# Splitting weights inside the attention loops: an edit of load order, waits and TensorE's tile order

## The reference, cut to what matters

```python
# 1: q, k, v [2, 8, 768, 64]; chunks of 32 queries, 16 keys to the left, 8 to the right, 8 memory keys
for c in range(nc):
    k_full = np.concatenate([mem_k, k_ctx], axis=2)
    scores = scale * np.matmul(q_c, k_full.transpose(0, 1, 3, 2))
    scores = scores - np.max(scores, axis=-1, keepdims=True)
    a = np.exp(scores)
    a = a / (np.sum(a, axis=-1, keepdims=True) + 1e-09)
    out[:, :, c_start:c_end] = np.matmul(a, v_full)
# 2: mix, x [2, 768, 512], w_k [512, 1024], w_v [1024, 512], w_r [512, 512]
xk = mu_k * x + (1.0 - mu_k) * x_prev
xr = mu_r * x + (1.0 - mu_r) * x_prev
k = np.maximum(xk @ w_k, 0.0)
v = k * k @ w_v
x = v / (1.0 + np.exp(-(xr @ w_r)))
# 3: each token goes to one of 8 experts, chosen by its own logits or by the token before it
h = np.maximum(x[b, s] @ w1[e], 0.0)
out[b, s] = p[e] * (h @ w2[e])
```

## Time and profile before

| | |
|---|---|
| median of three runs | 531.41 us (528.64 to 531.82) |
| the profiled execution, its own time | 533.26 us |
| its span | 531.5 us |
| TensorE busy, matmuls | 440.0 us, 83% |
| TensorE busy, weight loads | 366.4 us, 69% |
| VectorE busy | 245.9 us, 46% |
| ScalarE busy | 212.7 us, 40% |
| GpSimd busy | 55.3 us, 10% |
| chain that ended last | PE 67%, DMA 14%, issue 7%, DVE 5%, POOL 3%, ACT 2% |
| first mix matmul | 82.91 us |

### The profile page before, as it was taken

How to read it: one execution, slowest core, us unless ns; L and a number is a source line. 1 busy time by engine, 2 the same in 40 slices (tenths; PEclk the granted TensorE clock), 3 DMA queues, 4 the chain that set the end, 5 groups by cost and what they waited for, 6 DMA issues and landing times.

```text
span 531.5 us, 10141 instructions
## 1 busy us (share of the span) xinstructions
PE 440.0 (83%) x3759; PEld 366.4 (69%) x3759; DVE 245.9 (46%) x477; ACT 212.7 (40%) x319; POOL 55.3 (10%) x62
## 2 busy tenths in 40 slices
PE   1667628999999999999940069999999999999993
PEld 1545518889898989989830047777777777777772
DVE  2454575653535234354045149222382247464861
ACT  1333474663435253344022038222462245555750
POOL 0000000010100101010003601111111111111110
PEclk9967867999999999999975569999999999999998
DMA  8668442428000000000004779511173128383810
GB/s 302 253 208 294 157 181 86 152 90 309 0 0 0 0 0 0 0 0 1 2 0 158 238 281 406 209 54 40 52 227 136 40 71 253 141 251 132 271 61 10
DMA packets 18313, 67.31 MB, mean 127 GB/s; under 512 B 2734, under 2 KB 2734, under 8 KB 18288
## 3 DMA queue, kind: packets, MB, share of 16 engines
q1 hardware_dynamic: 13104, 50.92, 27.9%
q0 software_dynamic: 4896, 16.05, 8.8%
q10 hardware_dynamic: 288, 0.02, 0.0%
HBM read 55.41 MB, written 12.62 MB: 128 GB/s over the span
## 4 chain that ended last, share of the span: by engine, by line
PE 67%; DMA 14%; issue 7%; DVE 5%; POOL 3%; ACT 2%; SPq 1%; POOLq 0%; DVEq 0%; ACTq 0%
PE PS L530 16%; PE PS L403 12%; PE PS L513 12%; PE PS L435 10%; DMA QK<-tiles 5%; PE PS L419 5%; DMA XR<-grouped_rows 5%; POOL grouped_rows L1107 2%; PE PS L521 2%; PE PS L453 2%; PE PS L504 1%; PE PS L330 1%; PE PS L357 1%; DMA RAW<-wmix 1%; PE PS L343 1%
## 5 line engine op out<-in xcount | busy, mean ns | idle before, releaser
L1022 DVE TENSOR_TENSOR ELO<-ERAW,EHI 128x1024 fp32r<-128x1024 f32 x56 | 66.8, 1219 | 12.9 <-ACT EHI L696 10.3
L696 ACT ACTIVATE EHI<-ERAW 128x1024 fp32r<-128x1024 f32 x56 | 57.4, 1053 | 29.6 <-DMA ERAW<-wexp 20.8
L403 PE MATMUL PS<-XHI,WHI 128*128 128x256 f32 x192 | 56.6, 295 | 1.2 <-DVE WLO L805 1.2
L530 PE MATMUL PS<-EHI,HH 128*128 128x512 f32 x128 | 54.6, 426 | 2.6 <-issue 1.0
L403 PE MATMUL PS<-XHI,WLO 128*128 128x256 f32 x192 | 55.2, 287 | 0.0
L403 PE MATMUL PS<-XLO,WHI 128*128 128x256 f32 x192 | 55.1, 287 | 0.0
L513 PE MATMUL PS<-EHI,XSH 128*128 128x512 f32 x128 | 53.0, 414 | 1.4 <-DVE XSL L1030 1.4
L1043 DVE TENSOR_TENSOR HL<-PS,HH 128x512 fp32r<-128x512 f32 x32 | 22.1, 691 | 66.3 <-ACT HH L716 65.9
L513 PE MATMUL PS<-ELO,XSH 128*128 128x512 f32 x128 | 51.5, 402 | 0.0
L513 PE MATMUL PS<-EHI,XSL 128*128 128x512 f32 x128 | 51.2, 400 | 0.0
L530 PE MATMUL PS<-EHI,HL 128*128 128x512 f32 x128 | 50.6, 395 | 0.0
(11 more groups left out here) (141 smaller groups left out, 774.6 us busy)
## 6 DMA issues: line engine op xcount, KB each, us to landing
ERAW<-wexp SPq DMA_DIRECT2D x56, 512.0 KB, 5.6
QK<-tiles SPq DMA_DIRECT2D x12, 768.0 KB, 5.7
VV<-tiles SPq DMA_DIRECT2D x12, 520.0 KB, 3.9
grouped_rows<-ZR POOLq DMA_DIRECT2D x1, 5140.0 KB, 18.1
RAW<-wmix SPq DMA_DIRECT2D x10, 512.0 KB, 3.8
XR<-grouped_rows POOLq DMA_DIRECT2D x17, 257.0 KB, 4.2
CO<-consts SPq DMA_DIRECT2D x1, 470.0 KB, 6.5
rows_out<-OSB,OIDX POOLq DMA_INDIRECT x16, 3.9
```

What stands on the lines that cost most here:

```text
L403: last = nc.tensor.matmul(PS[q % 2][:, half * 256:half * 256 + 256], w[:, c:c + P], x[:, k, :], start=n == 0, stop=n == 11)
L530: last = nc.tensor.matmul(PS[4][:, :], x[:, f, :], ww[:, c:c + D], start=n == 0, stop=n == 23)
L696: nc.scalar.activation(EHI[w][:, c * CH2:(c + 1) * CH2], ERAW[c][:], ACT.Copy).then_inc(ehi_done, 1)
L1022: nc.vector.tensor_tensor(ELO[w][:, c * CH2:(c + 1) * CH2], ERAW[c][:], EHI[w][:, c * CH2:(c + 1) * CH2].bitcast(F32), ALU.subtract).then_ ...
```

## The change

All ten chunks are loaded, and split, inside the attention loops: SP loads chunk t at the end of `ahead(t)`, behind the QK load of tile t+4 and a wait for `weight_lo` of chunk t-2 (`wlo_done` starts at 2, so that the first two don't wait and every later count is higher by 2). ScalarE does `weight_hi(t-2)` at the end of tile step t, VectorE `weight_lo(t-2)` behind `normed(t)`, in all pairs but the first. The mix layer holds none of them any more.

The waits for the V and QK loads move from `probs_transposed` to `values` and `scores`. TensorE's tile order becomes probabilities(t), x(t-1), values(t), scores(t+2). Each of the two gets an increment of a semaphore, `passed_pe`, that no engine waits for.

`CO` is loaded in two parts: the identity where the whole was loaded, the tables behind the last chunk, with a semaphore of their own; `X2R`'s token column is filled from them in mix pair 0.

```diff
-            sp.dma_start(CO[:], consts).then_inc(const_in, 16)
+            sp.dma_start(CO[:, 0:C_LT], consts[:, 0:C_LT]).then_inc(const_in, 16)
...
-            def ahead(t, u, more=True):
+            def raw_next(n, u):
+                sp.wait_ge(wlo_done, n + 1)
+                raw_load(n, u)
+
+            def ahead(t, u):
                 sp.wait_ge(pv_done, t + 1)
                 v_load(t + 2, u)
-                if more:
-                    sp.wait_ge(scores_done, t + 3)
-                    qk_load(t + 4, u)
+                sp.wait_ge(scores_done, t + 3)
+                qk_load(t + 4, u)
+                raw_next(t, u)
...
-            ahead(NT - 4, 0, False)
-            ahead(NT - 3, 1, False)
-            for n in range(N1):
-                if n >= 2:
-                    sp.wait_ge(wlo_done, n - 1)
-                raw_load(n, n % 2)
+            for u in range(2):
+                sp.wait_ge(pv_done, NT - 3 + u)
+                v_load(NT - 2 + u, u)
+                raw_next(N1 - 2 + u, u)
+            sp.dma_start(CO[:, C_LT:CW], consts[:, C_LT:CW]).then_inc(tables_in, 16)
# TensorE
-            def scores(t, u, first):
-                pe.wait_ge(const_in, 48)
+            def scores(t, u, first, loads=16):
                 if first:
                     pe.wait_ge(qk_loaded[u], 16)
                 else:
                     pe.wait_ge(sub_done, t - 1)
+                    pe.wait_ge(qk_loaded[u], loads)
+                    pe.sem_inc(passed_pe, 1)
...
             def probs_transposed(t, u, first, more):
                 pe.wait_ge(exp_done, t + 1)
-                pe.wait_ge(v_loaded[u], 8 * (t - u) + 16)
-                if more:
-                    pe.wait_ge(qk_loaded[u], 8 * (t + 2 - u) + 16)
...
-            def values(t, u, first):
-                pe.wait_ge(const_in, 48)
+            def values(t, u, first, loads):
                 pe.wait_ge(pt_evac, t + 1)
+                pe.wait_ge(v_loaded[u], loads)
                 if not first:
                     pe.wait_ge(norm_done, t)
+                pe.sem_inc(passed_pe, 1)
...
             def attention(g, first, last):
+                loads = 16 * g + 16
+                ahead = 16 * g + 32
                 for u in range(2):
                     t = 2 * g + u
                     probs_transposed(t, u, first and u == 0, not last)
-                    if not last:
-                        scores(t + 2, u, False)
                     if not (first and u == 0):
                         x_transposed(t - 1, 1 - u, first and u == 1)
-                    values(t, u, first and u == 0)
+                    values(t, u, first and u == 0, loads)
+                    if not last:
+                        scores(t + 2, u, False, ahead)
# ScalarE, attention; VectorE has the same with weight_lo
-                    if last:
-                        for n in (2 * u, 2 * u + 1):
-                            weight_hi(n)
+                    if not first:
+                        weight_hi(t - 2, u)
# ScalarE, mix; VectorE has the same with weight_lo
-                    if first:
-                        weight_hi(N1A + q - 1)
                     relu_square(g, q, first)
-                if first:
-                    for n in range(N1A + 3, N1):
-                        weight_hi(n)
```

More of the change, by code:

```diff
@@ L35 @@
 QW, KW, VWT = HP * P, HP * CPT * KEYS, HP * CPT * VW
-INW = QW + KW + VWT
+QKW = QW + KW
+INW = QKW + VWT
 NPAIR = NT // 2
@@ L120, in moe_program @@
         inner = top[0]
-        QK = [place(f"QK{i}", [P, QW + KW]) for i in range(2)]
+        QK = [place(f"QK{i}", [P, QKW]) for i in range(2)]
         VV = [place(f"VV{i}", [P, VWT]) for i in range(2)]
@@ L157, in moe_program @@
         const_in = sem("const_in")
+        tables_in = sem("tables_in")
+        passed_pe = sem("passed_pe")
         qk_loaded = [sem(f"qk_loaded{i}") for i in range(2)]
@@ L245, in qk_load @@
             def qk_load(t, u):
-                sp.dma_start(QK[u][:], tiles[ds(t, 1), :, 0:QW + KW].rearrange("a p n -> (a p) n")
+                sp.dma_start(QK[u][:], tiles[ds(t, 1), :, 0:QKW].rearrange("a p n -> (a p) n")
                              ).then_inc(qk_loaded[u], 16)
             def v_load(t, u):
-                sp.dma_start(VV[u][:], tiles[ds(t, 1), :, QW + KW:INW].rearrange("a p n -> (a p) n")
+                sp.dma_start(VV[u][:], tiles[ds(t, 1), :, QKW:INW].rearrange("a p n -> (a p) n")
                              ).then_inc(v_loaded[u], 16)
@@ L385, in _ @@
             x_transposed(NT - 1, 1, False)
-            pe.wait_ge(wlo_done, N1A)
+            pe.wait_ge(wlo_done, N1A + 2)
             pe.wait_ge(xt_evac, NT)
@@ L410, in gate @@
                 if first:
-                    pe.wait_ge(wlo_done, N1A + KT * D // CH1)
+                    pe.wait_ge(wlo_done, N1A + KT * D // CH1 + 2)
                 else:
@@ L431, in down @@
                     if first and c % CH1 == 0:
-                        pe.wait_ge(wlo_done, c // CH1 + 1)
+                        pe.wait_ge(wlo_done, c // CH1 + 3)
                     r = slice(u * P, u * P + P)
@@ L479, in _ @@
             logits(NT - 1, 1)
+            pe.wait_ge(tables_in, 16)
             pe.wait_ge(route_step, R_FLAGS)
@@ L584, in x_out, with weight_hi @@
                                      ACT.Copy).then_inc(xt_evac, 1)
-            def weight_hi(n):
-                act.wait_ge(raw_loaded[n % 2], 16 * (n // 2 + 1))
-                nc.scalar.activation(WHI[:, n * CH1:(n + 1) * CH1], RAW[n % 2][:],
+            def weight_hi(n, u):
+                act.wait_ge(const_in, 48)
+                act.wait_ge(raw_loaded[u], 8 * (n - u) + 16)
+                nc.scalar.activation(WHI[:, ds(n * CH1, CH1)], RAW[u][:],
                                      ACT.Copy).then_inc(whi_done, 1)
@@ L800, in normed, with weight_lo @@
                 last.then_inc(norm_done, 1)
-            def weight_lo(n):
+            def weight_lo(n, u):
+                dve.wait_ge(const_in, 48)
                 dve.wait_ge(whi_done, n + 1)
-                c = slice(n * CH1, (n + 1) * CH1)
-                nc.vector.tensor_tensor(WLO[:, c], RAW[n % 2][:], WHI[:, c].bitcast(F32),
+                nc.vector.tensor_tensor(WLO[:, ds(n * CH1, CH1)], RAW[u][:], WHI[:, ds(n * CH1, CH1)].bitcast(F32),
                                         ALU.subtract).then_inc(wlo_done, 1)
@@ L828, in attention @@
                     normed(t, u, first)
-                    if last:
-                        for n in (2 * u, 2 * u + 1):
-                            weight_lo(n)
+                    if not first:
+                        weight_lo(t - 2, u)
                     if last and u == 0:
@@ L839, in _ @@
             nc.vector.tensor_scalar(OM[:], MU[:], -1.0, 1.0, ALU.mult, ALU.add)
-            nc.vector.tensor_copy(X2R[:, :, D + 1], CO[:, C_TOK:C_TOK + NT])
             nc.vector.memset(ZR[:, 0:D + 1], 0.0)
@@ L847, in _ @@
             dve.wait_ge(setup_done, 1)
+            dve.sem_inc(wlo_done, 2)
             shifted(0, 0, True)
@@ L881, in mix @@
                     logits_out(2 * g - 2)
-                if first:
-                    weight_lo(N1A)
                 squared(g, 1, first)
@@ L886, in mix @@
                     logits_out(2 * g - 1)
-                else:
-                    weight_lo(N1A + 1)
                 squared(g, 2, first)
                 if first:
-                    weight_lo(N1A + 2)
+                    dve.wait_ge(tables_in, 16)
+                    nc.vector.tensor_copy(X2R[:, :, D + 1], CO[:, C_TOK:C_TOK + NT])
                 squared(g, 3, first)
-                if first:
-                    for n in range(N1A + 3, N1):
-                        weight_lo(n)
                 if not last:
```

## The result

The changed kernel takes 534.5 us (median of 20 executions, 531.6 to 540.1) against 531.7 us for the kernel before (20 executions, 528.6 to 533.6). The ratio is **1.005, interval 1.0035 to 1.0066**: slower by 1.9 to 3.5 us, about half of the 1% named as the bound. Forecast were +1.9 us and "within 1%". The profiled execution took 534.89 us, its span is 533.1 against 531.5 us before.

What follows compares the result with a forecast made beforehand. The attention loop was taken as bound by latency, TensorE carrying most of the chain. Tail +2.4, mix pair 0 -1.0 and increments +0.5 gave +1.9 us: 535.2 against the profiled 533.26, 533.4 as median; range 527.5 to 539.

Steps and rivals of the forecast that it cites:

- The wait changes hands: Attention loop: TensorE's waits for QK loads go, and x transposes wait about 2 us a tile for VectorE's norm instead.
- Two chains of one length: Attention loop, after scores end: x transposes can start 2.95 us later behind VectorE's norm; ScalarE's probability copy ends 3.85 later.
- Start: Start of the kernel: with fewer constants ahead, first scores up to 1.0 us earlier than 7.88; scores(2) end at 15.9.
- Loop: Attention loop, scores(2) to scores(11): 52.6 us, later tiles 5.6 us at full clock, 6.3 at half; end at 68.4.
- the share of the lower clock: Attention loop: about 42% at the lower clock level, taken from the old loop's granted clock of 0.79.
- Tail: From the end of scores(11) to the first mix matmul: 16.95 us, so mix starts at 85.35, 2.4 later than before.
- Mix pair 0: First mix pair: waits of about 0.3 us for the last chunk and 0.66 for X2F go, -1.0 us.
- Increments: TensorE, two a tile, 20 in all, against two removed constant waits: 0 to 2.0 us, 0.5 taken.
- stayed low: Rival, TensorE in the loop: low clock throughout, mix at 89.7, +6.3 us, 537.7 us; chance 0.2.
- stayed high: Rival, TensorE in the loop: clock high throughout, mix at 82.2, -1.2 us, 530.2 us; chance 0.15.
- VectorE and ScalarE keep up: Rival, attention loop: the norm wait doesn't appear, tiles take 4.5 to 5.2 us, 521.3 to 527.6 us in all; chance 0.13.
- Loads were not late: Rival, loop loads: a chunk ahead of each QK and V load makes them late, 6 us more, 539 us; chance 0.05.

## Why the prediction was right

- *The wait changes hands.* Right, place and size: 17.8 us behind the norm, about 2 us in each of nine tiles; shown by both versions with the old order and by the one with the new order alone.
- *Two chains of one length.* Right: x 2.99 after the scores (2.95), the copy ready 66.34 - 62.57 = 3.77 after them (3.85), and the version with VectorE's chain turned waits for ScalarE's.
- *Start.* Mis-sized: scores(2) ended at 13.49 + 1.18 = 14.67, forecast 15.9. I let the gate weights' 5.5 us set the start. With 64 KB of constants instead of 470 the gate weights themselves landed in 4.2 us, the constants in 4.5, and everything was there at 5.9.
- *Loop.* From there to the end of scores(11), 68.61, it took 53.9 us, forecast 52.6. The term that failed is the share of the lower clock, taken over from the old loop as 42%; a clock of 0.68 means 64%, and with that the forecast's own tiles give 2 x 5.90 + 7 x 6.05 = 54.1. The bounds, 49.6 to 56.7, held it. Start and loop miss in opposite ways, by 1.2 and 1.4 us: that the first mix matmul was forecast at 85.35 and came at 85.51 is in part luck. (Two sums of the prediction are 0.1 off: 14.8 + 1.19 is 16.0, and 15.9 + 10.4 + 39.2 is 65.5.)
- *Tail.* 85.51 - 68.61 = 16.9, forecast 16.95.
- *Mix pair 0.* 1.0 us gained from the first mix matmul to the end, forecast 1.0. Up to the X2F transposes it is 1.7 (31.2 to 29.4), and 0.7 of it is lost again behind them, for a reason that I haven't found; so the size is partly luck. In nine versions with the weights in the loop the kernel takes 446.0 to 448.0 us behind the first mix matmul, in the five without 447.8 to 449.5.
- *Increments.* The forecast counted 20, there are 22. 0.5 us was too little if the first 22 cost what the second do, 2.5 us. But the loop with its measured clock has no room for that (54.1 by the sum, 53.9 measured, increments included), so the term is neither shown nor refuted.
- *Rivals.* The clock neither stayed low nor high. By the Trainium skill, "TensorE: Matmul & The Clock Gate", section "HAM oscillation — how this bites in real kernels", as the prediction quotes it, it should have stayed high, as the long load waits went. It fell to 0.68 with no wait in the loop over 2.3 us, so the trace doesn't agree. That VectorE and ScalarE keep up didn't happen in this order; with the old one they do, at 5.15, 4.64 and 4.47 us a tile, that rival's numbers. Loads were not late here: QK took 6.2 us of the 10 it had.

In the profile the sum is +1.6 us (533.1 against 531.5), in the medians +2.8; +1.9 was forecast.

Left open: what one of the first 22 increments costs, why 0.7 us are lost behind the X2F transposes, and whether the early identity lasts to the end of the kernel.

## What to carry to other kernels

A wait that goes and an order that comes with it can cancel out: price each alone. Change the order of one in-order engine only with the order of those that feed it, and before believing that one chain is the brake, add up the others from the same starting point; if two end together, removing either brings nothing. Here the waits at their own matmuls gave 1.1% alone, and the order that came with them cost more than that.

## What the runs showed of the hardware that I had not expected

- Work that leads to nothing can pay: six extra transposes a tile raised the mean granted clock of 20 to 60 us from 0.68 to 0.91.
- An added increment on TensorE cost about 0.11 us of the chain (2.5 us for 22, from one profile of each version; by the ratios 3.8 us).
- In four versions with the old tile order, those that wait least for QK as they come into the hardware loop (at most 1.8 us), TensorE stood still there in the middle of a group of 64 matmuls between which there is no wait, once in the values and once in the scores. The rows are those of the old tile order with the QK load first; with `weight_hi` early as well the halts are 2.91 and 3.78 us, with the weights left where they were 2.02 and 2.18, and with the QK load behind the V load 1.12 and 1.32. On the pace, taken from tile 5 on, they have no effect:

```profile
21.59 0.30 PE L363 MATMUL PS<-VV,PTS 64*32 64x65 f32 x4
...
24.58 0.96 PE L363 MATMUL PS<-VV,PTS 64*32 64x65 f32 x60 [2.69 <-issue]
...
26.51 1.17 PE L338 MATMUL PS<-QK 64*32 64x64 f32 x62
...
30.38 0.37 PE L338 MATMUL PS<-QK 64*32 64x64 f32 x2 [2.70 <-issue]
```

The transfers' share was 1.01 in 22 to 26 us. The profile's DMA view has a queue named "instruction", with few transfers of 16 KB. In this version one goes from 22.30 to 23.36 and one from 28.08 to 29.12, inside the two halts, and in all eight halts the matmuls go on 1.2 to 1.5 us after such a transfer has ended; so they do in two short ones, 0.20 and 0.25 us, of versions with the new order. In the changed kernel they start at 20.54 and 26.16, where TensorE comes to wait for the norm anyway (x at 23.48 and 29.20), and there is no halt. So TensorE waiting for its own instructions behind the data fits all of this; that it is the cause is argued and not shown, since no run moves these transfers alone.
